# One-hot marks with the slot ahead of the tile, in 2 bytes, and a first list made by VectorE alone

## The reference

```python
attn_out = _attn_ref(q, k, v, n_global, n_local)        # 4 x 8 heads, 768 x 64, local window
x = attn_out.transpose(0, 2, 1, 3).reshape(3072, 512)
x = (silu(x @ w_in)) @ w_out                            # 512 -> 2048 -> 512
# third stage: routing with capacity, then 8 experts
logits = x @ w_gate                                     # (3072, 8)
flat = logits.flatten(); order = np.argsort(-flat)      # all (token, expert) pairs, best first
for idx in order:
    tok, e = idx // E, idx % E
    if assigned[tok] >= 0 or counts[e] >= cap: continue # cap = 3072 / 8 = 384
    assigned[tok] = e; counts[e] += 1
for e in range(E):
    mask = assigned == e
    out[mask] = np.maximum(x[mask] @ w1[e], 0.0) @ w2[e]
```

## Time and profile before

| | us |
|---|---|
| median of three runs (lowest, highest) | 1111.2 (1108.63, 1112.04) |
| profiled execution, its own time | 1112.91 |
| span of the profiled core | 1111.3 |
| PE busy | 1059.1 (95% of the span) |
| VectorE (DVE) busy | 630.0 (57%) |
| ScalarE (ACT) busy | 456.1 (41%) |
| POOL busy | 422.3 (38%) |
| mean granted TensorE clock | 0.978 of full speed |

### The profile page before, as it was taken

One profiled execution on the slowest core, in us unless ns is written; L12 is line 12 of the kernel. 1 busy time (PEld: TensorE's weight loads), 2 busy tenths in 40 slices (PEclk: granted clock), 3 DMA queues, 4 the chain that ended last, 5 costly groups with the idle time before them and its releaser, 6 DMA issues. The chain is left out here.

```text
span 1111.3 us, 21228 instructions
## 1 busy us (share of the span) xinstructions
PE 1059.1 (95%) x8004; PEld 907.6 (82%) x8004; DVE 630.0 (57%) x2219; ACT 456.1 (41%) x1167; POOL 422.3 (38%) x472
## 2 busy tenths in 40 slices
PE   7799999999999999999999999939999999999998
PEld 5587888888888888888888889828777877878987
DVE  6844747475656566565656553366766766756210
ACT  3664444444444444444444432203233323233442
POOL 1243222222222222222222223217477557486873
PEclk8999999999999999999999999959999999999999
DMA  6563212111212121211121000005225334323420
GB/s 202 192 211 125 74 54 73 55 66 52 73 54 73 55 73 55 72 51 60 49 70 54 30 11 20 2 19 180 97 113 199 115 134 142 133 106 127 196 104 29
DMA packets 19145, 99.99 MB, mean 90 GB/s; under 512 B 2800, under 2 KB 2800, under 8 KB 16848
## 3 DMA queue, kind: packets, MB, share of 16 engines
q0 software_dynamic: 9824, 58.99, 15.1%
q1 hardware_dynamic: 9216, 39.61, 10.6%
HBM read 86.00 MB, written 12.85 MB: 89 GB/s over the span
## 5 line engine op out<-in xcount | busy, mean ns | idle before, releaser
L382 POOL TENSOR_TENSOR g_low<-g,g_high 128x256 fp32r<-128x256 f32 x192 | 152.7, 796 | 469.3 <-ACT g_high L586 469.1
L480 PE MATMUL up_ps<-x_high,w_high 128*128 128x256 f32 x768 | 227.8, 297 | 4.5 <-DVE g L733 4.5
L480 PE MATMUL up_ps<-x_low,w_high 128*128 128x256 f32 x768 | 216.5, 282 | 0.0
L480 PE MATMUL up_ps<-x_high,w_low 128*128 128x256 f32 x768 | 216.3, 282 | 0.0
L733 DVE SCALAR_TENSOR_TENSOR g<-g,up_ps 128x256 f32<-128x256 f32 x192 | 80.3, 418 | 208.0 <-ACT g L579 208.0
L586 ACT ACTIVATE g_high<-g 128x256 fp32r<-128x256 f32 x192 | 80.2, 418 | 230.4 <-PE down_ps L493 125.5
L480 PEld LDWEIGHTS up_ps<-x_high,w_high 128*128 128x128 f32 x768 | 145.2, 189 | 15.6 <-issue 7.7
L493 PE MATMUL down_ps<-w_high,g_high 128*128 128x512 f32 x384 | 152.5, 397 | 0.0
L493 PE MATMUL down_ps<-w_low,g_high 128*128 128x512 f32 x384 | 152.0, 396 | 0.0
L493 PE MATMUL down_ps<-w_high,g_low 128*128 128x512 f32 x384 | 151.9, 396 | 0.0
L480 PEld LDWEIGHTS up_ps<-x_low,w_high 128*128 128x128 f32 x768 | 145.4, 189 | 2.9
(11 more groups left out here) (202 smaller groups left out, 1870.5 us busy)
## 6 DMA issues: line engine op xcount, KB each, us to landing
qk_t<-qk_rows SPq DMA_DIRECT2D x24, 720.0 KB, 4.3
v_w<-v_win SPq DMA_DIRECT2D x24, 464.0 KB
w_raw<-weights SPq DMA_DIRECT2D x16, 512.0 KB, 7.3
x_rest<-x_any POOLq DMA_DIRECT2D x24, 256.0 KB, 3.0
x_rows<-x POOLq DMA_DIRECT2D x12, 512.0 KB, 3.2
w_raw<-gate_rows SPq DMA_DIRECT2D x1, 2048.0 KB, 6.9
x_g<-x_rows,token_index POOLq DMA_INDIRECT x24, 3.6
out<-y,token_index POOLq DMA_INDIRECT x24, 2.7
```

Of the source, the lines that this page charges most:

```text
L382: pool.tensor_tensor(g_low[:, u % 2, :], g[:, u % 2, :], g_high[:, u % 2, :].bitcast(F32), ALU.subtract)\
L480: last = nc.tensor.matmul(up_ps[:, u % 2, 0:GT * P], a[:, f, w], x[:, grp % 2, c, :], start=k == 0, stop=k == 3 * C - 1)
```

## The change

The one-hot tile becomes `[P, P, T]`: the slot is the outer index and the tile the inner one, so that the 128 weights of a tile lie 24 elements (48 bytes) apart. A tile `slots` of the same shape holds the slot numbers in 2 bytes, repeated for each of the 24 tiles; ScalarE writes it once, when the numbers are there (`numbers_known`, `slots_made`). Round 0's `modulo` goes to a 2-byte tile in SBUF, `modulo_first`; that of the later rounds stays in PSUM in 4 bytes. POOL's part of round 0 is gone with `modulo_kept`, and VectorE makes all four quarters of it.

```diff
--- before.py
+++ after.py
@@ -1018,14 +1018,16 @@
         first = sb("first", [P, T])
         spare = sb("spare", [P, T])
         now_kept = sb("now_kept", [P, T])
+        modulo_first = sb("modulo_first", [P, T], BF16)
         newly = sb("newly", [P, T])
         taken = sb("taken", [P, 2, T], BF16)
         scan = sb("scan", [P, 2 * T])
         past_one = sb("past_one", [P, T])
         third = sb("third", [P, T, CT])
-        modulo_kept = sb("modulo_kept", [P, T // QUARTERS])
         ids = sb("ids", [P, T, 2, CT], BF16)
-        one_hot = sb("one_hot", [P, T, P], BF16)
+
+        one_hot = sb("one_hot", [P, P, T], BF16)
+        slots = sb("slots", [P, P, T], BF16)
         token_index = sb("token_index", [P, E, CT], I32)
         weight_index = sb("weight_index", [P, E, 1], I32)
 
@@ -1055,8 +1057,8 @@
             notes_used[0] += columns
             return notes_ps[:, notes_used[0] - columns:notes_used[0]]
 
-        (best, rank, key, over, dead, assigned, second, spare_note, chosen, own_chosen, base_chosen, now, third_of,
-         modulo) = (note(T) for _ in range(14))
+        (best, rank, key, over, dead, assigned, second, spare_note, chosen, own_chosen, base_chosen, now,
+         third_of, modulo) = (note(T) for _ in range(14))
         bits = note(T).bitcast(I32)
         place = note(2 * T).rearrange("p (k t) -> p k t", k=2)
         closed, won_note, first_wins = note(E), note(E), note(E)
@@ -1083,8 +1085,8 @@
         wins_counted = sem("wins_counted")
         weight_index_ready = sem("weight_index_ready")
         marks_ready = sem("marks_ready")
-        modulo_known = sem("modulo_known")
-        last_quarter_ready = sem("last_quarter_ready")
+        numbers_known = sem("numbers_known")
+        slots_made = sem("slots_made")
         marks_summed = sem("marks_summed")
         one_hot_ready = sem("one_hot_ready")
         listed = sem("listed")
@@ -1229,17 +1231,7 @@
                         out=out_rows, out_offset=bass.IndirectOffsetOnAxis(ap=token_index[:, p, t:t + 1], axis=0),
                         in_=y[:, par, t, :], in_offset=None).then_inc(y_stored[par], 16)
 
-            def mark_last_places():
-
-
-                pool.wait_ge(modulo_known, 1)
-                for t in range(T // QUARTERS):
-                    last = pool.tensor_scalar(one_hot[:, T - T // QUARTERS + t, :], row_s, modulo_kept[:, t:t + 1], None,
-                                              ALU.is_equal)
-                last.then_inc(last_quarter_ready, 1)
-
             fetch_w1(0)
-            mark_last_places()
             fetch_tokens(0)
             fetch_w2(0)
             rest_w1(0)
@@ -1287,13 +1279,11 @@
             def list_tokens(r):
                 for t in range(T):
                     quarter = t // (T // QUARTERS)
-                    if r == 0 and t == (QUARTERS - 1) * (T // QUARTERS):
-                        pe.wait_ge(last_quarter_ready, 1)
-                    elif r == 0 and t % (T // QUARTERS) == 0:
+                    if r == 0 and t % (T // QUARTERS) == 0:
                         pe.wait_ge(one_hot_ready, quarter + 1)
                     elif t == 0:
-                        pe.wait_ge(one_hot_ready, (r + 1) * QUARTERS - 1)
-                    last = nc.tensor.matmul(tokens_at, one_hot[:, t, :], ids[:, t, :, :].rearrange("p k c -> p (k c)"),
+                        pe.wait_ge(one_hot_ready, (r + 1) * QUARTERS)
+                    last = nc.tensor.matmul(tokens_at, one_hot[:, :, t], ids[:, t, :, :].rearrange("p k c -> p (k c)"),
                                             start=t == 0, stop=t == T - 1)
                 last.then_inc(listed, 1)
 
@@ -1423,6 +1413,9 @@
                 act.wait_ge(expert_down, p * CT + t + 1)
                 nc.scalar.activation(y[:, p % 2, t, :], down_ps[:, t, :], ACT.Copy).then_inc(y_ready, 1)
 
+            act.wait_ge(numbers_known, 1)
+            nc.scalar.activation(slots[:, :, :], row_s.unsqueeze(2).broadcast_to([P, P, T]), ACT.Copy)\
+                .then_inc(slots_made, 1)
             for f in range(FC):
                 round_w1(0, f)
             for p in range(E):
@@ -1465,7 +1458,8 @@
                 v.memset(a[:, :], 0.0)
             v.memset(places[:, :], float(CAP)).then_inc(places_known, 1)
             dve.wait_ge(numbers_made, 1)
-            link(v.tensor_copy(numbers[:, :], ints[:, :]))
+            v.tensor_copy(numbers[:, :], ints[:, :]).then_inc(numbers_known, 1)
+            dve.wait_ge(numbers_known, 1)
             link(v.tensor_copy(first_wins, first_wins_made))
 
             def wanted(r):
@@ -1584,11 +1578,9 @@
                 link(v.tensor_scalar(past_one[:, :], now[:, :], float(P), None, ALU.is_ge))
                 v.tensor_tensor(base_chosen[:, :], chosen[:, :], tile_base, ALU.mult)
                 link(v.scalar_tensor_tensor(third_of[:, :], now[:, :], float(2 * P), past_one[:, :], ALU.is_ge, ALU.add))
-                if r == 0:
-                    last_t = slice(T - T // QUARTERS, T)
-                    v.scalar_tensor_tensor(modulo_kept[:, :], third_of[:, last_t], -float(P), now_kept[:, last_t],
-                                           ALU.mult, ALU.add).then_inc(modulo_known, 1)
-                v.scalar_tensor_tensor(modulo[:, :], third_of[:, :], -float(P), now_kept[:, :], ALU.mult, ALU.add)
+
+                v.scalar_tensor_tensor(modulo_first[:, :] if r == 0 else modulo, third_of, -float(P), now_kept[:, :],
+                                       ALU.mult, ALU.add)
                 link(v.tensor_tensor(third[:, :, :], third_of[:, :].unsqueeze(2).broadcast_to([P, T, CT]),
                                      row_s[:, 0:CT].unsqueeze(1).broadcast_to([P, T, CT]), ALU.is_equal))
                 for k, of in enumerate((base_chosen, own_chosen)):
@@ -1598,8 +1590,10 @@
             def mark_places(r, quarter):
 
                 at_t = slice(quarter * T // QUARTERS, (quarter + 1) * T // QUARTERS)
-                v.tensor_tensor(one_hot[:, at_t, :], row_s.unsqueeze(1).broadcast_to([P, T // QUARTERS, P]),
-                                modulo[:, at_t].unsqueeze(2).broadcast_to([P, T // QUARTERS, P]), ALU.is_equal)\
+                if (r, quarter) == (0, 0):
+                    dve.wait_ge(slots_made, 1)
+                v.tensor_tensor(one_hot[:, :, at_t], slots[:, :, at_t],
+                                (modulo if r else modulo_first)[:, at_t].unsqueeze(1).broadcast_to([P, P, T // QUARTERS]), ALU.is_equal)\
                     .then_inc(one_hot_ready, 1)
 
             def keep_list(r):
@@ -1626,8 +1620,7 @@
                 elif k == SUMS:
                     list_them(r)
                 elif k < LIST:
-                    if (r, k) != (0, LIST - 1):
-                        mark_places(r, k - MARK)
+                    mark_places(r, k - MARK)
                 else:
                     keep_list(r)
                     if r + 1 < E - 1:
```

## The result

The changed kernel took 1123.4 us (median of 4 runs, 1119.61 to 1124.43) against 1110.07 us for the kernel before (4 runs, 1108.63 to 1112.04; three of them are the runs timed ahead of the prediction). The recorded ratio is 1.0085, 95% interval 1.0061 to 1.0109, which is 9.4 us (6.8 to 12.1). The two medians are further apart, 13.3 us or 1.2%, and nothing recorded says where the rest of that lies; what follows explains the 9.9 us between the two profiled executions. All of these say slower. The forecast was no change, 1111.6 us, with a range up to 1118. The profiled execution of the changed kernel took 1122.81 us, its span is 1121.2 us, 9.9 us longer than before.

The account below looks back on a forecast made before the run. PE, busy for 95% of the span, was taken as the bound. Four terms of 0 and 0.4 us for the loads gave 1113.3 us for the profiled execution, a median of 1111.6 us, range 1108 to 1118 us.

Parts of the forecast that it names:

- Round 0, marks: First list: VectorE's four quarters, at double rate, end at 754.8 us, before the unread products end at 756.00: 0 us.
- Round 0, POOL: First list: POOL loses six marks of 3.53 us in all, but its next work waits for `token_index`: 0 us.
- ScalarE: Writing `slots` once, about 2.7 us between 726 and 729 us, hidden well ahead of its reader: 0 us.
- Later marks: Rounds 1 to 7: 28 quarters on VectorE stay at 945 ns, with no gain from 2-byte slots: 0 us.
- Rival 2: VectorE's marks in later rounds get faster through 2-byte slots: up to 4 us less, 1107.2 us; chance 0.08.
- rival 4: The new layout slows VectorE's marks, 2.1 us in round 0 and 3.6 us later: 1117 us; chance 0.06.
- All rounds, weight loads: PE's 192 list loads, weights now 48 bytes apart, cost 2 ns more each: 0.4 us, bounds 0 to 17 us.
- rival 3: List loads: each weight costs its own access, up to 17 us, 1128 us; half hidden 9 us, 1120 us; chance 0.09.
- Rival 1: List loads on PE lose their double rate, pitch 47 ns for 25: 4.2 us slower, 1115.4 us; chance 0.15.

Follow-up runs that it names:

- probe: Kernel before, its 17 unread products behind the first list replaced by unread loads at steps of 2 to 48 bytes: 1134.83 us, 25.0 to 67.9 ns per load.
- e2: Changed kernel without the step: one-hot tile and slots laid out with the tile ahead of the slot as before; 1117.69 us, ratio 0.9991 to the kernel before.
- s2: Changed kernel with the one-hot tile in twelve groups of two tiles, weights 4 bytes apart; 1117.88 us, ratio 0.9995 to the kernel before.
- e3: Kernel before with weights 48 bytes apart and VectorE's marks in the changed kernel's order, from the old 4-byte operands; 1126.84 us, ratio 1.0089.
- s6: Changed kernel with the one-hot tile in four groups of six tiles, weights 12 bytes apart; 1123.79 us, ratio 1.0041 to the kernel before.
- s2_fewer_unread: Changed kernel with weights 4 bytes apart and 8 in place of 10 unread products ahead of the first list; 1117.16 us, ratio 0.9985 to the kernel before.

## Why the prediction was wrong

Point by point, by its own steps.

- *Round 0, marks*: 0, and right. The unread products did hide them. One reading there was loose: the clock of 0.50 was read for all 6.26 us of these products, but its row ends at 752 us, and the clock rose near 755.5. The marks started at 753.82 us (752.91 before, in a trace that is 0.97 us earlier there), took 2.06 us (576 ns each, forecast 546) and ended at 755.88, 1.1 us ahead of the unread products.
- *Round 0, POOL*: 0, right; POOL idled 7.6 us there, until `token_index`.
- *ScalarE*: one instruction of 2.76 us at 727.0, forecast 2.7; its reader came at 753.8.
- *Later marks*: 947 ns, forecast 945. Rival 2 (a gain by type) and rival 4 (dearer marks) fall with this.
- *All rounds, weight loads*: this step failed. It put 2 ns on a load, 0.4 us in all; the load took 42.9 ns more, 8.2 us. The 2 ns came from the row of 31 columns beside that of 128: equal length was taken as slack before a slower read is seen. The slack is small: it holds for 4 bytes and is used up at 8, and at 48 bytes a list of 24 loads spans 1.63 us in place of the 0.60 to 0.65 forecast. The probe shows what that row can't: 128 columns take 25 to 68 ns, and up to a step of 16 bytes the time follows the number of 16-byte lines that they lie in, 16 for 128 packed weights and 128 for these. The one stepped read in the trace, VectorE's at 16 bytes and 0.70 ns per element, was set aside as another engine's. It would have been the better guide: the load grew from 96 to 176 ns, 0.63 ns per weight, and half of that reached the pitch.
- *The rivals*: rival 3, each weight an access of its own, half hidden, had 9 us and 1120 us, with a chance of 0.09 and outside the range. It comes nearest in mechanism, with 128 lines for 128 weights. That its size was near is in part luck: the price per element was VectorE's, and no row gave the half. Rival 1 (the loss of a double rate, 22 ns) fell with the free step of 4 bytes, where two weights no longer touch. Its 22 ns were also misread: the 53 ns of the matmul were taken off a pitch of 100 ns as if load and matmul followed each other, and the probe shows them side by side. The measured 8.2 us lies within the bounds that the prediction gave this term, 0 to 17 us; the faults were the choice within them, and a range that left out the upper part of the only term without a row of its own.

Settled by runs: without the step between the weights the loss is gone (e2, s2), with the step alone it is there (e3), and a cheaper step costs less (s6). The price of a load follows the number of lines from 8 to 16 bytes (probe). Argued only: that the load reads the lines one by one. Open: the 9 ns from 16 to 48 bytes, why the clock drops where it does, whether the step adds to the drops, and the 4 us between the 9.4 us of the recorded ratio and the 13.3 us of the medians.

No version was shown faster than the kernel before. s2_fewer_unread comes nearest, 0.9985 with an interval that just holds 1. By their ratios to the kernel before it beats the changed kernel, whose interval begins at 1.0061; the two weren't run side by side.

## What to carry to other kernels

When a layout is turned to help the engine that writes a tile, look up who reads it, and price the read in 16-byte lines: a stationary operand whose 2-byte weights lie 16 bytes or more apart cost 59 to 68 ns per 128 of them here. Six moving columns hid almost nothing of that; beside 128 of them a step of 48 bytes cost 13 ns more than one of 12. Take the smallest inner group that keeps the writer's pair together; two 2-byte elements kept VectorE's double rate (552 ns for 947) and the load's 25 ns. An operation that no row shows is to be priced by the nearest row of its kind of access, on whatever engine, before the nearest row of its kind of instruction.

## What was not expected of the hardware

- VectorE's writes of 2 bytes, each to a new 16-byte line (48 bytes apart), took 3.9 us per 768 elements against 0.945 in runs of six and 1.03 at 4 bytes; POOL's 1.10 us per 128 against 0.59 in order and 0.63 at 4 bytes.
- The time of a stepped weight load is the same at both levels of TensorE's clock: 46.3 ns (lower) and 45.8 ns (full) at 12 bytes, 67.9 ns on both at 48. At 4 bytes it was 28.3 ns at the lower level and 25.0 ns at the full one.
- A VectorE instruction with both inputs in SBUF stood 7.27 us behind POOL's back-to-back work.
